# Splitting q, k and v by pairs of heads on GpSimd with copies by DMA, blocks without padding, and the value product in two halves of 288

## What is computed

```python
scores = scale * q @ k.T                       # 4 x 8 heads, 576 x 576, head_dim 64
cum    = cumsum(max(s, 0))                     # per head
bias   = min(-(cum[:, None] - cum[None, :]), 0)
attn   = softmax(where(causal, -1e9, scores + bias))
x      = (attn @ v) as (2304, 512)
h  = x @ w_in                                  # (2304, 1024)
ln = layernorm(h * softmax(h)) * g_ln
x2 = ln @ w_out                                # (2304, 512)
y  = max(x2 @ w1, x2 @ w2, x2 @ w3) @ w_out2   # inner 768, output (2304, 512)
```

## Time and profile before

| | us |
|---|---|
| median of 3 runs (lowest, highest) | 772.84 (771.74, 778.02) |
| profiled execution | 775.42 |
| its span in the profile | 773.3 |
| busy in the span: TensorE, VectorE, ScalarE, GpSimd | 727.6, 418.7, 328.3, 225.7 |

### The profile page before, as it was taken

The page is one execution under the profiler, slowest core; times in us unless marked ns, Lnnn a source line. Parts: engine busy times, 40 slices in busy tenths (PEclk is TensorE's granted clock), DMA queues, the critical chain, the costliest instruction groups (busy, mean ns, idle before and its releaser), DMA issues.

```text
span 773.3 us, 12787 instructions
## 1 busy us (share of the span) xinstructions
PE 727.6 (94%) x4312; PEld 662.6 (86%) x4312; DVE 418.7 (54%) x766; ACT 328.3 (42%) x795; POOL 225.7 (29%) x240
## 2 busy tenths in 40 slices
PE   3898999899899899999999999999999999999997
PEld 2777788788787788989898989999989999899995
DVE  8999999999985675535444364513203123032120
ACT  2888888888784443423233243412112121121111
POOL 6756669878762631404040200000000000000000
PEclk9999999999999999999999999999999999999999
DMA  6465464545341110106100031000010000100101
GB/s 154 115 165 139 135 149 119 131 124 143 88 91 43 42 37 6 41 1 176 29 0 0 0 109 56 1 21 22 1 42 1 14 28 0 41 0 0 41 0 42
DMA packets 46580, 45.28 MB, mean 59 GB/s; under 512 B 22164, under 2 KB 37652, under 8 KB 46516
## 3 DMA queue, kind: packets, MB, share of 16 engines
q1 hardware_dynamic: 46548, 44.86, 22.2%
HBM read 39.43 MB, written 5.38 MB: 58 GB/s over the span
## 4 chain that ended last, share of the span: by engine, by line
PE 66%; DMA 8%; POOL 7%; DVE 6%; issue 6%; SPq 4%; ACT 2%; POOLq 0%; ACTq 0%
PE ps L600 10%; PE ps L602 10%; PE ps L601 10%; DMA qk_raw<-in_qk_dram 8%; PE ps L532 4%; PE ps L534 4%; PE ps L533 4%; PE ps L520 4%; PE ps L522 4%; PE ps L521 4%; PE ps L613 3%; PE ps L614 3%; PE ps L615 3%; POOL qk_b L671 2%; POOL v_hl L675 2%
## 5 line engine op out<-in xcount | busy, mean ns | idle before, releaser
L602 PE MATMUL ps<-x_lo,w_hi 128*128 (+1 forms) x432 | 144.4, 334 | 0.0
L600 PE MATMUL ps<-x_hi,w_hi 128*128 128x384 f32 x432 | 144.3, 334 | 0.0
L601 PE MATMUL ps<-x_hi,w_lo 128*128 128x384 f32 x432 | 144.3, 334 | 0.0
L783 ACT ACTIVATE probs<-ps,nmax 128x576 f32<-128x576 f32 (+4 forms) x160 | 82.7, 532 | 14.2 <-DVE nmax L1002 14.2
L793 ACT ACTIVATE pt_hi<-ps 128x512 fp32r<-128x512 f32 (+1 forms) x128 | 69.7, 570 | 35.3 <-PE ps L432 32.6
L414 PE MATMUL ps<-k_a,q_a 128*128 128x288 f32 (+2 forms) x192 | 70.0, 369 | 12.9 <-DVE q_a L995 12.3
L432 PE MATMUL ps<-ident,probs 128*128 128x128 f32 x480 | 74.6, 285 | 7.7 <-DVE pt_lo L1009 3.1
L600 PEld LDWEIGHTS ps<-x_hi,w_hi 128*128 128x128 f32 x432 | 81.1, 188 | 0.2
L601 PEld LDWEIGHTS ps<-x_hi,w_lo 128*128 128x128 f32 x432 | 81.1, 188 | 0.2
L602 PEld LDWEIGHTS ps<-x_lo,w_hi 128*128 128x128 f32 x432 | 81.1, 188 | 0.0
L1009 DVE TENSOR_TENSOR pt_lo<-ps,pt_hi 128x512 fp32r<-128x512 f32 (+1 forms) x128 | 77.9, 649 | 3.4 <-ACT pt_hi L793 2.2
(11 more groups left out here) (102 smaller groups left out, 1469.1 us busy)
## 6 DMA issues: line engine op xcount, KB each, us to landing
qk_raw<-in_qk_dram SPq DMA_DIRECT2D x64, 288.0 KB, 4.3
rinvB<-rsum_dram SPq DMA_DIRECT2D x24, 192.0 KB, 4.0
stage<-in_moe_w_dram SPq DMA_DIRECT2D x18, 256.0 KB, 4.2
out_dram<-stage SPq DMA_DIRECT2D x18, 256.0 KB, 2.0
v_raw<-in_v_dram SPq DMA_DIRECT2D x32, 128.0 KB, 2.4
stage<-in_moe_w_out_dram SPq DMA_DIRECT2D x14, 256.0 KB, 2.7
stage<-in_moe_w_in_dram SPq DMA_DIRECT2D x4, 512.0 KB, 3.3
aux_dram<-setup SPq DMA_DIRECT2D x1, 576.0 KB, 4.6
```

Of the source, the lines that this page charges most:

```text
L600: pe.matmul(dst, w_hi[f][:, i, c, :], x2_hi[par][:, c, :], start=(c == 0), stop=False)
L601: pe.matmul(dst, w_lo[f][:, i, c, :], x2_hi[par][:, c, :], start=False, stop=False)
L602: mm = pe.matmul(dst, w_hi[f][:, i, c, :], x2_lo[:, c, bass.ds(g * GT, GT)], start=False, stop=(c == KC - 1))
L783: act.activation(dst, SCORES[c], ACT.Exp, bias=nmax[par][:, c:c + 1], accum_out=sums_all[:, c, bass.ds(t, 1)]).then_inc(exp_done, 1)
```

## The change

- The row blocks are 64, 128, 128, 128, 128 queries, without padding (first_of). So the zeroing of the padding goes, block 0 of scores and of the transposes works on 64 rows.
- q and k of two heads are loaded by one DMA of 128 partitions into `split`, two pairs ahead. GpSimd makes there, for both heads at once, the scaled q, the high parts and the low parts (in place). Three DMAs for each head copy them into `oper` (k_a, q_a, q_b, k_b of a head; two buffers, one for each parity): copy_high, copy_low. With aux that makes 64 counts of oper_loaded a head, and TensorE's scores 4 wait for them instead of the four counts of GpSimd and VectorE.
- q's low part leaves VectorE, v's high part goes from ScalarE to GpSimd. For the first pair of heads, k's parts are made by GpSimd, q's high part by ScalarE and q's low part by VectorE after the running sums.
- The value product is cut at 288 columns in both banks; ScalarE copies both low halves by one instruction (copy_vlo, after PV_B), VectorE adds both by one (add_parts, where add_a stood). PV_A waits for x_done of head t-3.
- TensorE waits for all pt_lo of the slot before ahead of scores 0, not ahead of turn 1.

```diff
+def first_of(c):
+    return 0 if c == 0 else P * c - P // 2
...
-    J2, J0, J1, J4, J3, TW = 0, 3 * P, 8 * P, 12 * P, 13 * P, 15 * P
+    J2, J0, J1, J4, J3 = 0, 3 * P, 3 * P + S, 7 * P + S, 8 * P + S
+    TW = J3 + 2 * P
     GROUPS = [
         ([(2, 2), (2, 3), (2, 4), (0, 0)], J2),
-        ([(0, 1), (0, 2), (0, 3), (0, 4)], J0 + P),
+        ([(0, 1), (0, 2), (0, 3), (0, 4)], J0 + PAD),
         ([(1, 1), (1, 2), (1, 3), (1, 4)], J1),
         ([(4, 4), (3, 3), (3, 4)], J4),
     ]
     GBANK = [3, 4, 3, 4]
...
-    PV_A = [(0, J0 + PAD, J0 + 3 * P, 0), (1, J1, J1 + 2 * P, PAD), (2, J2, J2 + P, PAD + P)]
-    PV_B = [(0, J0 + 3 * P, J0 + 5 * P, 0), (1, J1 + 2 * P, J1 + 4 * P, 0), (2, J2 + P, J2 + 3 * P, 0),
-            (3, J3, J3 + 2 * P, 0), (4, J4, J4 + P, P)]
+    GCOLS = [3 * P + PAD, 4 * P, 4 * P, 3 * P]
+    GROWS = [P, P - PAD, P, P]
+    PV_A = [(0, J0, J0 + HALF, 0), (1, J1, J1 + HALF - PAD, PAD), (2, J2, J2 + HALF - P - PAD, P + PAD)]
+    PV_B = [(0, J0 + HALF, J0 + S, 0), (1, J1 + HALF - PAD, J1 + 4 * P, 0), (2, J2 + HALF - P - PAD, J2 + 3 * P, 0),
+            (3, J3, J3 + 2 * P, HALF - 2 * P), (4, J4, J4 + P, HALF - P)]
...
+            split_t = sb(a, "split", [P, 2, 4, ROW])
...
-            vlo_a = sb(a, "vlo_a", [D, QA])
-            vlo_b = sb(a, "vlo_b", [D, QB])
...
-            q_a = [sb(a, f"q_a{i}", [P, SP], F32R) for i in range(2)]
-            qk_b = [sb(a, f"qk_b{i}", [P, SP + S], F32R) for i in range(2)]
-            k_a = [sb(a, f"k_a{i}", [P, S], F32R) for i in range(2)]
+            vlo = sb(a, "vlo", [D, 2, HALF])
...
+            oper_t = [sb(a, f"oper{i}", [P, 4, ROW], F32R) for i in range(2)]
...
-            def load_qk(h, par):
-                rows = qkT[bass.ds(h, 1)].rearrange("a d i s -> (a d) (i s)")
-                for copy in range(2):
-                    dst = qk_raw[par][D * copy:D * (copy + 1), :, :].rearrange("p i s -> p (i s)")
-                    sp.dma_start(dst, rows).then_inc(qk_loaded[par], 16)
+            def load_qk(pair, pb):
+                sp.dma_start(split[:, pb, 2:4, :], qkT[bass.ds(pair, 1)].rearrange("a p i s -> (a p) i s")).then_inc(qk_loaded[pb], 16)
...
+            def copy_high(h, pb):
+                rows = slice(D * h, D * (h + 1))
+                sp.dma_start(f32(oper[h][0:D, 0:2, :]), split[rows, pb, 0:2, :]).then_inc(oper_loaded[h], 16)
+            def copy_low(h, pb):
+                rows = slice(D * h, D * (h + 1))
+                sp.dma_start(f32(oper[h][D:P, 0:2, :]), split[rows, pb, 0:4:3, :]).then_inc(oper_loaded[h], 16)
+                sp.dma_start(f32(oper[h][0:D, 2:4, :]), split[rows, pb, 1:3, :]).then_inc(oper_loaded[h], 16)
...
             load_qk(0, 0)
+            load_qk(1, 1)
             load_v(0, 0)
-            load_qk(1, 1)
-            sp.wait_ge(rows_zeroed, 2)
+            load_v(1, 1)
+            sp.wait_ge(k0_hi_ready, 1)
+            sp.wait_ge(q0_hi_ready, 1)
+            copy_high(0, 0)
+            sp.wait_ge(k0_lo_ready, 1)
+            sp.wait_ge(q0_lo_ready, 1)
+            copy_low(0, 0)
             sp.wait_ge(cum_ready, 1)
             for h in range(2):
-                rows = setup[h:h + 1, :, :].rearrange("a (r i) s -> a r (i s)", i=2)
-                sp.dma_start(f32(qk_b[h][D:D + 4, PAD:SP + S]), rows).then_inc(aux_loaded[h], 16)
+                rows = setup[h:h + 1, :, :].rearrange("a (r i) s -> a r i s", i=2)
+                sp.dma_start(f32(oper[h][D:D + 4, 2:4, :]), rows).then_inc(oper_loaded[h], 16)
+            copy_high(1, 0)
+            copy_low(1, 0)
             sp.dma_start(aux_dram, setup[:, :, :]).then_inc(aux_stored, 16)
             sp.dma_start(g_sb[:, :], g_ln).then_inc(g_loaded, 16)
...
+            def reload_qk(pair, pb):
+                sp.wait_ge(oper_loaded[0], pair * 64 - 64)
+                sp.wait_ge(oper_loaded[1], pair * 64 - 64)
+                load_qk(pair, pb)
+            def refill(pair, h, pb):
+                t = 2 * pair + h
+                if h == 0:
+                    sp.wait_ge(lo_ready, pair)
+                    sp.sem_inc(sp_passed, 1)
+                sp.wait_ge(scores_done, 3 * (t - 1))
+                copy_high(h, pb)
+                copy_low(h, pb)
+                load_aux(t, h)
+            def reload_v(h, par):
+                sp.wait_ge(v_lo_ready, h - 1)
+                load_v(h, par)
+            def reload_pair(pair, pb, known=None):
+                if known is None or known + 2 < PAIRS:
+                    reload_qk(pair + 2, pb)
+                if known == 0:
                     sp.wait_ge(aux_stored, 16)
-                sp.wait_ge(scores_done, 3 * (t - 1))
-                load_aux(t, par)
...
+                refill(pair + 1, 0, 1 - pb)
+                if known != 0:
+                    reload_v(2 * pair + 1, 1)
+                refill(pair + 1, 1, 1 - pb)
+                reload_v(2 * pair + 2, 0)
+            reload_pair(0, 0, 0)
+            reload_pair(1, 1, 1)
...
-                cols = slice(P * c, P * (c + 1))
+                cols = slice(first_of(c), first_of(c + 1))
                 pe.matmul(o, q_a[par][:, cols], k_a[par][:, k0:k1], start=True, stop=False)
-                mm = pe.matmul(o, q_b[par][:, cols], k_b[par][:, k0:k1], start=False, stop=(m0 is None))
+                mm = pe.matmul(o, q_b[par][0:D + 4, cols], k_b[par][0:D + 4, k0:k1], start=False, stop=(m0 is None))
                 if m0 is not None:
-                    w = PAD if c == 0 else P
-                    mm = pe.matmul(o[:, m0:m0 + w], ident_b[:, :], mask[:, P - w:P], start=False, stop=True)
+                    w = first_of(c + 1) - first_of(c)
+                    mm = pe.matmul(o[:, m0:m0 + w], ident_b[:, 0:w], mask[:, 0:w], start=False, stop=True)
...
                 for n, (j, c) in enumerate(blocks):
-                    o = chunk_offset(c) + P * j
-                    mm = pe.transpose(ps[:, GBANK[g], P * n:P * (n + 1)], probs[1 - par][:, o:o + P], ident[:, :])
+                    o = chunk_offset(c) + first_of(j)
+                    q = first_of(c + 1) - first_of(c)
+                    k = P if c == 0 else first_of(j + 1) - first_of(j)
+                    mm = pe.transpose(ps[0:k, GBANK[g], P * n:P * n + q], probs[1 - par][0:q, o:o + k], ident[0:q, 0:q])
                 mm.then_inc(turned, 1)
...
-                pe.wait_ge(aux_loaded[par], (t - par) * 8 + 16)
+                pe.wait_ge(oper_loaded[par], (t - par) * 32 + 64)
                 if known != 0:
...
                     score_pass(SCORES[3], 0, 4 * P - PAD, 3, par, 3 * P - PAD)
+                    if live(known, 1) and known != 1:
+                        pe.wait_ge(pt_lo_done, 4 * (t - 1))
                     score_pass(SCORES[0], 0, P - PAD, 0, par, 0).then_inc(scores_done, 1)
+                elif live(known, 1):
+                    pe.wait_ge(pt_lo_done, 4 * (t - 1))
                 if live(known, 1):
...
                     if known != 2:
-                        pe.wait_ge(xa_done, t - 2)
+                        pe.wait_ge(x_done, t - 2)
...
                 if live(known, 2):
-                    if known != 2:
-                        pe.wait_ge(xb_done, t - 2)
...
+            def scale_q(pair, pb):
+                pool.wait_ge(qk_loaded[pb], (pair - pb) * 8 + 16)
+                pool.sem_inc(pool_passed, 1)
+                q = split[:, pb, 3, :]
+                pool.tensor_scalar(q, q, SCALE, 1.0, ALU.mult, ALU.mult).then_inc(q_scaled, 1)
+            def qk_high(pair, pb):
+                pool.wait_ge(q_scaled, pair)
+                pool.sem_inc(pool_passed, 1)
+                pool.tensor_scalar(split[:, pb, 0:2, :].bitcast(F32R), split[:, pb, 2:4, :], 1.0, 1.0, ALU.mult,
+                                   ALU.mult).then_inc(hi_ready, 1)
+            def qk_low(pair, pb):
+                pool.wait_ge(hi_ready, pair)
+                raw = split[:, pb, 2:4, :]
+                pool.tensor_tensor(raw.bitcast(F32R), raw, split[:, pb, 0:2, :], ALU.subtract).then_inc(lo_ready, 1)
...
+            def split_v(h, par, known):
+                pool.wait_ge(v_loaded[par], (h - par) * 16 + 32)
                 if known is None or known >= 2:
-                    pool.wait_ge(scores_done, 3 * (t - 1))
+                    pool.wait_ge(pv_done, 2 * (h - 1))
                 pool.sem_inc(pool_passed, 1)
...
-            def split_v(h, par):
+                pool.tensor_scalar(v_hl[par][:, :, 0:D], v_raw[par][:, :, :], 1.0, 1.0, ALU.mult, ALU.mult).then_inc(v_hi_ready, 1)
                 pool.wait_ge(v_hi_ready, h + 1)
                 pool.tensor_tensor(v_hl[par][:, :, D:2 * D], v_raw[par][:, :, :], f32(v_hl[par][:, :, 0:D]),
                                    ALU.subtract).then_inc(v_lo_ready, 1)
...
+            k0_hi, k0 = split[:, 0, 0, :], split[:, 0, 2, :]
+            pool.wait_ge(qk_loaded[0], 16)
+            pool.tensor_scalar(k0_hi.bitcast(F32R), k0, 1.0, 1.0, ALU.mult, ALU.mult).then_inc(k0_hi_ready, 1)
```

(52 more changed lines are left out.)

227 lines of the change are left out of this document (81 added, 146 removed).

## The result

The changed kernel takes 833.22 us (median of 4 runs, 825.40 to 833.73), the kernel before 773.19 beside it: a ratio of 1.0744, 95% interval 1.0677 to 1.0811. That is slower, 60 us off the forecast and 44 above the range. The profiled execution took 833.73 with a span of 831.9, 58.6 more than the span before.

What follows compares the result with a forecast made beforehand. Bound: a ring through TensorE, VectorE, TensorE, ScalarE, 6.68 us a slot against 6.80. Over 25 slots -3.0, start +2.7, end +0.4 give +0.1, carried to the median as 773.0 us; range 766 to 789.

Steps and rivals of the forecast that it cites:

- landed 6.5 to 7 us after the start, in time by some 2 us, so nothing is added: Copies of a head's operands into oper: would land within the 8.6 us available, adding nothing to the slot.
- The prediction's own sign for it: If landings rule, TensorE's first score of a head waits for a DMA into oper, with DMA share near 1.
- SP issues at 0.59 a DMA: four are out after 2.4 us: SP's issuing of a head's three copies and aux: 0.59 us each, 2.4 us for the four.
- The copies' own time: Data time of one head's copies inside SBUF: taken as 4.0 us, with 2.4 to 7.7 considered.
- the queue's total: DMA work for a pair of heads: 11.9 of 13.4 us, a share of 0.89.
- rival (a): DMA queue becomes the bound if a head's copies (c) take above 4.7 us: 790 us; chance 0.19.
- far end of 844: DMA queue as bound with a head's copies at 7.7 us: a pair takes 19.3 us, +71, 844 us.
- 64 instead of 128 rows: TensorE's block 0 turns and scores: -0.03 us a slot, up to 0.1; value product unchanged within 0.1.
- The merged addition: VectorE's single 64x576 addition before the value product: 0.772 us (0.70 to 0.85), adding 0.29 to every slot.
- VectorE emptied: q's low part leaves VectorE, which then idles until row block 0's scores: leg 1 shortens only from 2.20 to 2.10 us.
- rival (b): VectorE's load was the bound, so slots fall to TensorE's own 6.25 us: 762 us; chance 0.07.
- The start: Before the first score: split and copies delay it from 12.29 to 15.5 us; +2.7 us taken (1 to 5).

Runs made afterwards that it cites:

- experiment 4: Changed kernel with v of each head loaded by ScalarE's queue in that head's own slot instead of by SP: 810.87 us.
- experiment 8: Kernel before without padding and with the merged addition, plus one TensorE wait for three small chained DMAs: 800.21 us, 11.0 above the same kernel without the stall.
- experiment 9: Kernel before with only the merged value product, copy and addition: 779.31 us; kernel before with only the padding taken out: 789.13 us, ratio 1.0216.
- experiment 11: Kernel before with VectorE's first addition moved ahead of row maxima 0 and 3: 768.15 us, ratio 0.9921; with the merged addition as well: 770.53 us.
- experiment 1: Kernel before with no padding, halves of 288, one copy and one addition, q and k split and loaded as before: 789.22 us, ratio 1.0164.
- experiment 5: Changed kernel loading only 64 of every 512 columns of w_in and w_out, the others zeroed: 815.03 us.

## Why the prediction was wrong

**The step that failed** is "landed 6.5 to 7 us after the start, in time by some 2 us, so nothing is added". Head 8's refill landed 11.8 us after its start, heads 12's and 14's 10.1 and 11.3. The prediction's own sign for it was there: first scores that wait for a DMA into oper, at a share of 1.01. The start was not the trouble: it came 0.26 to 1.25 us after the scores that it waits for. I put 1.6 us of a q and k load ahead of the copies and no piece of w_in, and summed the queue as a mean over pairs. The expectation of experiment 4 (SP "runs a whole slot behind") comes from taking the refill of 73.57 for head 8's; it is head 9's. No run put the load of q and k behind the refill instead of ahead of it, which would test this account directly.

A smaller miss lies in the same passage: "SP issues at 0.59 a DMA: four are out after 2.4 us". The four of head 8 took 4.1 us (67.22 to 71.27) and v's two another 2: I carried over two issues that had no copies ahead of them. I never summed SP over a pair, which has 13 or 14 issues: at 0.59 that is 8 us, and it measured 11.5 of 14.5. SP had time left for 36.5 us of waits for scores, but it issued w_in and q and k late, close ahead of the refill; taking v off SP gave 22 us back.

**The copies' own time** was about right (4.0 forecast; 885 KB at 213 GB/s are an estimate of 4.2), and the queue's total was too small where it mattered. The 0.89 was a mean over pairs, with 0.7 for the weights; a pair with a piece of w_in moves 3.2 MB (2 x 0.88 copied, 0.59 q and k, 0.29 v, 0.52 w_in, 0.04 aux), at the 213 GB/s measured from 66 to 78 us 15.1 us for 14.4. The prediction's 231 came from a load. The page behind it, the Trainium skill, "SBUF — State Buffer", "Door 1: The DMA port swizzle", has 218 at most and 196 measured for 64 partitions; 213 lies between, and 231 (at a share of 1.04) above both, so "the trace's 231 agrees" was too kind. So rival (a), the queue as the bound, holds in part, in the four pairs with w_in, though c stayed under its 4.7; its price of 790 was too low, because it had no stall and no clock in it. (Its far end of 844 also leaves out the 3 us that its 790 has.)

**The price of a stall** had no place in the sum. The 9.2 us of waits came with 72 us at half clock, 29 us more by the estimate above. The one stall of experiment 8 shows it without the copies: 3.4 us cost 11.

**64 instead of 128 rows** was taken at -0.03 a slot, and the value product at nothing within 0.1. It cost 14.4 us (experiment 9): the second failed step, wrong in sign. Here the bound was not drawn from both sides, because no row of before had a 64-row matmul, and fewer columns looked like an end of the range.

**The merged addition** was right in kind: 0.74 for 0.772 forecast, +4.1 us alone where 0.29 a slot gave 7. In the changed kernel it mostly hides: TensorE waits 0.4 at most for it, where 0.6 to 0.8 in every slot was forecast.

**VectorE emptied**: as forecast, it idles until the score of row block 0, and nothing came of it. Its busy share fell from 96% to about 70% in stretches at full clock (50.04 of 71 us from 143 to 214), and no slot became shorter. Alone this would not refute rival (b), since TensorE's own work had grown; experiment 11 does more: with VectorE's work as before, its order alone gave 6.6 us, so its load was not what set the slot.

**The start** was forecast at +2.7, first score at 15.5; it came at 17.09 (12.29 before), behind the load of aux, and the first addition 9.4 late. A stretch of 7 us at half clock lies there too; so it does in the kernel of experiment 1, whose first addition is 4.5 late.

By runs, the 60 us are: 14 to 16 for the matmuls over 64 rows, addition included; 32 for late refills (issues and bytes, with the half clock that they bring); and some 12 for the later start, the remaining short waits and the spread of the runs (the changed kernel's own span from 825.40 to 833.73, and six of its variants ran once).

## What to carry to other kernels

Before you call a refill in time, add up what stands ahead of it in its queue at that moment, the largest piece included, and not the mean over a period: head 8's refill stood behind 1.1 MB of other loads. Find out which transfer a wait is for by counting the semaphore, and read its start and its landing apart. Sum the issuing engine too, and take the issue time from behind transfers of the same size, for there it measured 1.31 us where 0.59 was assumed. On an engine at full clock price a stall above its length, since the granted clock may halve behind it (here 3.4 us cost 11), and price an edit that puts 64-row matmuls between 128-row ones as a cost, not a gain. When one addition delays TensorE, look first at the order on the engine that makes it: moving it ahead of two instructions gave more than the whole change was to give.

## What the runs showed that was not expected

- How long the clock stays at half does not follow the length of the stall: 38 us behind an idle time of 1.01 (214.00, changed kernel), 27 behind 3.50, 7 behind 2.62, 13 behind 3.36 (experiment 8), 17 behind 1.49 (experiment 5). None behind 1.42 (145.23, the kernel before).
- A DMA of 18 KB issued behind three copies of 288 KB holds SP for 1.31 us, behind three of 144 KB for 0.74.
- Traffic of which about half is copies inside SBUF moved at 213 GB/s (66 to 78 us), near the 231 of loads: no sign that reading and writing share one path, which was the far end of the forecast (7.7 us a head).
